# Feed-forward token blocks of 256 columns in place of 512

## The reference, cut to what matters

```python
def _moe_ref(x, w_in, w_out):
    h = x @ w_in                                # 384 -> 2048
    g = h * (1.0 / (1.0 + np.exp(-1.702 * h)))
    return (g @ w_out).astype(np.float32)       # 2048 -> 384

def _moe2_ref(x, w_in, w_out):
    h = x @ w_in
    g = h - np.tanh(h)
    return (g @ w_out).astype(np.float32)

# reference: x is the attention's output as (3072, 384)
x = _moe_ref(x=x, **moe_kwargs)
return _moe2_ref(x=x, **moe2_kwargs)
```

## Time and profile before

| | us |
|---|---|
| median of 2 runs (1152.47 to 1153.01) | 1152.74 |
| the profiled execution | 1147.88 |
| its span, first to last instruction | 1146.1 |
| TensorE busy in the span | 1061.9 (93%) |
| DVE busy | 629.0 (55%) |
| ACT busy | 335.8 (29%) |
| POOL busy | 317.5 (28%) |

### The profile page before, as it was taken

The page is one execution under the profiler, slowest core; times in us unless marked ns, Lnnn a source line. Parts: engine busy times, 40 slices in busy tenths (PEclk is TensorE's granted clock), DMA queues, the critical chain, the costliest instruction groups (busy, mean ns, idle before and its releaser), DMA issues.

```text
span 1146.1 us, 23498 instructions
## 1 busy us (share of the span) xinstructions
PE 1061.9 (93%) x8640; PEld 913.5 (80%) x8640; DVE 629.0 (55%) x1906; ACT 335.8 (29%) x646; POOL 317.5 (28%) x460
## 2 busy tenths in 40 slices
PE   4878787888788999999999999999999999999997
PEld 4877777778787888888888888888888888888886
DVE  8999999999994433333333334333333334333332
ACT  0111111111114533333333335533333333333332
POOL 6677767776774510000000005510000000000000
PEclk9888888887888999999999999999999999999999
DMA  3222322322235500000000003300000000000000
GB/s 92 77 63 73 79 67 67 79 79 58 76 92 161 167 28 1 1 1 1 1 1 1 0 0 94 99 14 1 28 1 28 1 1 28 1 28 0 27 0 27
DMA packets 50717, 46.97 MB, mean 41 GB/s; under 512 B 24400, under 2 KB 46032, under 8 KB 50640
## 3 DMA queue, kind: packets, MB, share of 16 engines
q1 hardware_dynamic: 46544, 41.13, 12.7%
q10 hardware_dynamic: 4096, 4.72, 1.3%
HBM read 36.39 MB, written 9.44 MB: 40 GB/s over the span
## 4 chain that ended last, share of the span: by engine, by line
PE 81%; DVE 11%; issue 6%; DMA 1%; ACT 0%; SPq 0%; DVEq 0%; ACTq 0%; POOL 0%; POOLq 0%
PE bank L510 34%; PE bank L522 34%; DVE scores L791 4%; PE bank L455 4%; PE bank L421 2%; DVE sf L674 2%; PE bank L466 2%; PE bank L475 1%; PE bank L485 1%; PE bank L426 1%; DVE pf L674 1%; DVE t L674 1%; DVE k L733 1%; PE bank L440 1%; DVE sf L671 1%
## 5 line engine op out<-in xcount | busy, mean ns | idle before, releaser
L510 PE MATMUL bank<-x_hi,win_hi 128*128 128x512 f32 x576 | 225.4, 391 | 2.2 <-DVE x_lo L848 2.2
L510 PE MATMUL bank<-x_hi,win_lo 128*128 128x512 f32 x576 | 225.2, 391 | 0.0
L510 PE MATMUL bank<-x_lo,win_hi 128*128 128x512 f32 x576 | 225.0, 391 | 0.0
L522 PE MATMUL bank<-g_hi,wout_hi 128*128 128x512 f32 x576 | 224.3, 389 | 0.8 <-DVE g_lo L863 0.8
L522 PE MATMUL bank<-g_lo,wout_hi 128*128 128x512 f32 x576 | 224.1, 389 | 0.0
L522 PE MATMUL bank<-g_hi,wout_lo 128*128 128x512 f32 x576 | 224.1, 389 | 0.0
L863 DVE TENSOR_TENSOR g_lo<-g,g_hi 128x512 fp32r<-128x512 f32 x192 | 133.7, 696 | 134.2 <-ACT g_hi L634 134.2
L791 DVE COPY_PREDICATED scores<-mask,bank 128x144 f32<-128x144 int32 (+2 forms) x576 | 168.1, 292 | 3.1
L634 ACT ACTIVATE g_hi<-g 128x512 fp32r<-128x512 f32 x192 | 121.5, 633 | 149.4 <-DVE g L858 74.9
L860 DVE TENSOR_TENSOR g<-bank,sg 128x512 f32<-128x512 f32 x96 | 66.3, 691 | 176.4 <-ACT sg L630 176.4
L858 DVE TENSOR_TENSOR g<-bank,sg 128x512 f32<-128x512 f32 x96 | 66.3, 691 | 175.8 <-ACT sg L628 175.8
(11 more groups left out here) (60 smaller groups left out, 1334.3 us busy)
## 6 DMA issues: line engine op xcount, KB each, us to landing
w_raw<-w_in SPq DMA_DIRECT2D x32, 192.0 KB, 2.3
w_raw<-w_out SPq DMA_DIRECT2D x32, 192.0 KB, 2.5
alpha<-a_t SPq DMA_DIRECT2D x64, 72.0 KB, 2.1
r<-q_t SPq DMA_DIRECT2D x64, 72.0 KB, 2.3
k<-k_t SPq DMA_DIRECT2D x64, 72.0 KB, 2.1
v<-v_l SPq DMA_DIRECT2D x32, 144.0 KB, 2.2
attn_out<-y ACTq DMA_DIRECT2D x64, 72.0 KB, 2.0
x_all<-attn_out SPq DMA_DIRECT2D x6, 768.0 KB, 4.5
```

The source lines that it names most:

```text
L510: last = nc.tensor.matmul(pH[f % 2][:], win(w, f, m), x[xp][:, m, :], start=(n == 0), stop=(n == len(terms) - 1))
L522: last = nc.tensor.matmul(pO[m][:], wout(w, f, m), gp[f % 2][:], start=(f == 0 and n == 0), stop=(f == NF - 1 and n == 2))
```

## The change

The token block has 256 columns instead of 512, so there are twelve blocks per layer. Every tile of the feed-forward part that holds tokens is half as wide, and the PSUM tiles use the first half of their banks. The x loads follow the new number of blocks: block 1 is loaded after weight slice 2, block 2 after slice 3 and so on, blocks 10 and 11 after slice 11. Before, block 1 was loaded after slice 3, block 2 after slice 5 and so on.

```diff
@@ -66,7 +66,7 @@
-TB = 512
+TB = 256
 NT = TOK // TB
 TILES = NT * NF
@@ -165,8 +165,8 @@
-        pH = [bank[0], bank[1]]
-        pO = [bank[2 + m] for m in range(KC)]
+        pH = [bank[n][:, 0:TB] for n in range(2)]
+        pO = [bank[2 + m][:, 0:TB] for m in range(KC)]
@@ -222,9 +222,9 @@
             if m == 1:
-                nc.vector.tensor_copy(dst, pO[m][:]).then_inc(o_copied, 1)
+                nc.vector.tensor_copy(dst, pO[m]).then_inc(o_copied, 1)
             else:
-                nc.scalar.activation(dst, pO[m][:], ACT.Copy).then_inc(o_copied, 1)
+                nc.scalar.activation(dst, pO[m], ACT.Copy).then_inc(o_copied, 1)
@@ -298,8 +298,10 @@
             for F in range(2, NF):
                 for side in range(2):
                     load_slice(side, F)
-                if F % 2 and F // 2 < NT:
-                    load_x(F // 2)
+                if F < NT:
+                    load_x(F - 1)
+                if F == NT - 1:
+                    load_x(NT - 1)
@@ -507,7 +509,7 @@
-                    last = nc.tensor.matmul(pH[f % 2][:], win(w, f, m), x[xp][:, m, :],
+                    last = nc.tensor.matmul(pH[f % 2], win(w, f, m), x[xp][:, m, :],
...
```

More of the change, by code:

```diff
@@ L521, in down @@
                     for n, (w, gp) in enumerate(terms):
-                        last = nc.tensor.matmul(pO[m][:], wout(w, f, m), gp[f % 2][:],
+                        last = nc.tensor.matmul(pO[m], wout(w, f, m), gp[f % 2][:],
                                                 start=(f == 0 and n == 0), stop=(f == NF - 1 and n == 2))
@@ L627, in _ @@
                     if layer == 0:
-                        nc.scalar.activation(SG[f % 2][:], pH[f % 2][:], ACT.Sigmoid, scale=1.702).then_inc(sg_done, 1)
+                        nc.scalar.activation(SG[f % 2][:], pH[f % 2], ACT.Sigmoid, scale=1.702).then_inc(sg_done, 1)
                     else:
-                        nc.scalar.activation(SG[f % 2][:], pH[f % 2][:], ACT.Tanh).then_inc(sg_done, 1)
+                        nc.scalar.activation(SG[f % 2][:], pH[f % 2], ACT.Tanh).then_inc(sg_done, 1)
                     act.wait_ge(g_done, N + 1)
@@ L857, in _ @@
                     if layer == 0:
-                        nc.vector.tensor_tensor(G[f % 2][:], pH[f % 2][:], SG[f % 2][:], ALU.mult).then_inc(g_done, 1)
+                        nc.vector.tensor_tensor(G[f % 2][:], pH[f % 2], SG[f % 2][:], ALU.mult).then_inc(g_done, 1)
                     else:
-                        nc.vector.tensor_tensor(G[f % 2][:], pH[f % 2][:], SG[f % 2][:], ALU.subtract).then_inc(g_done, 1)
+                        nc.vector.tensor_tensor(G[f % 2][:], pH[f % 2], SG[f % 2][:], ALU.subtract).then_inc(g_done, 1)
                     dve.wait_ge(gh_done, N + 1)
```

## The result

The changed kernel takes 1219.76 us (two runs, 1219.54 to 1219.99) against 1152.74; the ratio is 1.0581, with a 95% interval of 1.0536 to 1.0627. The forecast was 1218 in a range from 1186 to 1254. The profiled execution took 1219.99, its span is 1217.8, against 1146.1 before: 71.7 us more.

The account below looks back on a forecast made before the run. TensorE alone was taken to set the pace, with over a microsecond of side-chain slack. 46.1 + 7.8 + 7.4 + 5.6 - 1.6 = +65.3 us on 1147.9, plus 4.9 to the median, gave 1218 us, range 1186 to 1254.

Parts of the forecast that it names:

- Step 1: Feed-forward matmuls on TensorE: one fixed gap of 13.3 ns each, so 120 ns at 256 columns, +46.1 us.
- rival A: The gap between matmuls scales with the columns: 113.3 ns each, 1189 us in all; chance 0.10.
- Rival B: Not slower: the gap vanishes at short lengths, only the load's 112 ns remains, 1153 us; chance 0.08.
- Step 2: Weight loads on TensorE: each holds the array 0.112 us, just below 0.120, and costs nothing.
- Rival C: Weight load and gap add: 125 ns per matmul, 1246 us in all; chance 0.12.
- Rival D: Loads don't overlap matmuls at this length: 0.218 us each, 1876 us in all; chance 0.03.
- Step 3: ACT and DVE side chain: remainder usable 2.12 us after the last up matmul starts; fits by 0.05 us.
- two-step rule: Two steps tied by the side chain last max(36 x 0.120, 2.23 + 17 x 0.120) = max(4.32, 4.27) us.
- Steps 4 and 5: Per block: x_lo makes product 7 late, +7.8 us; DVE's copy out of output banks delays slice 0, +7.4 us.
- Step 6: Weights being split, block 0 and last block of layer 1: 2.36 us a step against 2.16, +5.6 us.
- Step 7: Start about 1.6 us earlier, about 1.0 lost to slice 3 queued behind x, shorter end: together -1.6 us.

Follow-up runs that it names:

- experiment 10: Blocks of 128 columns, 24 per layer, x loads after the weights, otherwise the changed kernel: 3310.9 us (one run).
- experiment 5: Changed kernel (256 columns) with one more DVE operation of 192 columns before each product: 1264.5 us, ratio 1.100 to the kernel before.
- experiment 6: Kernel before (512 columns) with one more DVE operation of 192 columns before each product: 1152.9 us, ratio 1.003.
- experiment 1: Changed kernel with the split of the next block's x cut in thirds, at slices 6, 7 and 8: 1211.5 us, ratio 1.052 to the kernel before.
- experiment 2: Changed kernel with a second set of output banks for odd blocks: 1213.2 us, ratio 1.054 to the kernel before.
- experiment 3: Changed kernel with x of block 1 loaded after weight slice 3, blocks 2 to 11 after all layer 1 weights: 1211.6 us, ratio 1.052.

## Why the prediction was right, and where it was not

**Step 1, the matmul.** Right in size: 120.0 ns at 256 columns, and 173.3 at 384. The fixed gap is shown at three lengths, and rival A falls by them. One leg of the argument was wrong: attention's missing gap. Rows of the timeline at three moments within the twelve records of the earlier trace rows, each beginning with the oldest matmul that still runs:

```profile
204.67 0.57 PE L455 MATMUL bank<-r,k 48*64 48x160 f32 x5
...
204.71 0.53 PE L455 MATMUL bank<-r,k 48*64 48x160 f32 x4
...
204.81 0.47 PE L455 MATMUL bank<-r,k 48*64 48x160 f32 x4
```

The starts are 0.036 and 0.100 apart in turn. The two heads lie in two halves of the rows and run side by side, and one half has a matmul every 0.136 us: 0.85 ns per column, not 0.417. The 0.0667 was an average over both halves. These rows, which are also of another type, float32, said nothing of a float32r column or its gap. So they gave no ground for 120 over 113.3 ns, and that the choice came out right is partly luck. Rival B rested on the same rows.

**Step 2, the weight load.** Right: a load holds the array for 0.112 us (experiment 10), reading it from the two load starts after a stall was sound, and its record of 0.19 is not the price. Rival C (load and gap add) is refuted by 0.120. Rival D is refuted by the interval too: load and stream in series would be 0.218. The rule that the prediction quotes beside it from the Trainium skill, "TensorE: Matmul & The Clock Gate", Part 3, doesn't hold here: loads and matmuls on the same 128 rows start 0.12 apart throughout.

**Step 3, the side chain.** Right in kind and in size. The remainder ends 2.07 after the start of the last up matmul, and where a load waits for it, it starts 0.05 to 0.06 later (experiment 5: the remainder ends at 603.81, the load starts at 603.87), which makes 2.12, the forecast. The single lengths are off by up to 0.02 and cancel. Experiment 5 shows the two-step rule, experiment 6 that it has no force at 512.

**Steps 4 and 5, slices 7 and 0.** Right in place, releaser and size, and each removed alone (experiments 1 and 2).

**Step 6, the weight loop.** Right in size for layer 2's weights (2.4 for 2.8), but it had only half of the mechanism. It let POOL's operation be longer (1.1), and the trace shows that DVE's is too: of a POOL remainder and a DVE remainder in SBUF, the one that starts second takes up to the whole overlap longer. In block 0 of the changed kernel:

```profile
378.13 0.96 DVE L850 TENSOR_TENSOR x_lo<-x_all,x_hi 128x768 fp32r<-128x768 f32 x1 [0.31 <-ACT x_hi L618]
378.59 1.37 POOL L332 TENSOR_TENSOR win_lo<-w_raw,win_hi 128x384 fp32r<-128x384 f32 x1 [1.32 <-ACT win_hi L581]
...
382.04 1.01 POOL L332 TENSOR_TENSOR wout_lo<-w_raw,wout_hi 128x384 fp32r<-128x384 f32 x1
382.14 1.20 DVE L865 TENSOR_TENSOR g_lo<-g,g_hi 128x256 fp32r<-128x256 f32 x1 [0.48 <-ACT g_hi L636]
```

POOL takes 1.37 instead of 1.00 behind x_lo, and g_lo 1.20 instead of 0.43 behind POOL. So g_lo, the end of a chain without slack, is late in the steps in which weights are split. What share of the stalls of blocks 0, 11 and 12 this is, no run separates.

**Step 7, block 0 and the start: mis-sized.** "The six more x transfers (12 of half the size) pass before they are needed" looked at who needs x, not at who stands behind it. Issued one per slice in steps half as long, they double the rate at which x competes with the weights. I had 3.8 us with the weight loop; it was 10.8, and experiment 3 takes 8.3 off the 13.8. The start came out 1.4 us late instead of 1.6 early: 2.2 because attention itself ended later in this execution, and x_lo of block 0 took 1.67 us in place of 0.96. The first is chance: over all kept profiles the last attention matmul starts between 349.5 and 355.8, in code that no edit touched. The second is POOL, which had begun a remainder first, as in step 6; experiments 2, 3 and 5, which have the same overlap, have the same 1.67:

```profile
352.78 0.99 POOL L332 TENSOR_TENSOR wout_lo<-w_raw,wout_hi 128x384 fp32r<-128x384 f32 x1
...
352.92 1.67 DVE L850 TENSOR_TENSOR x_lo<-x_all,x_hi 128x768 fp32r<-128x768 f32 x1 [0.56 <-ACT x_hi L618]
```

**The sum and the hit.** The sum was 6.4 us short in the span, and the distance of 4.9 us between the profiled execution and the median of before, which I added to it, filled most of that: after the change the two coincide. So that the forecast missed by only 1.7 us is partly luck; the terms together are good to about 6 us, of which 2.2 is the chance end of attention. The distance itself was chance too: the later runs of the kernel before have medians of 1149.7 to 1150.9, 2 to 3 us below the 1152.7 that it was taken from.

## What to carry to other kernels

Before halving a matmul, count three prices: the gap that comes with each one, the time a weight load holds the array (from two load starts after a stall, not from the record's length), and the slack of the chain of other engines, which doesn't halve, since ACT and DVE operations keep a fixed part (here 0.38 to 0.43 us each at 256 columns, 0.60 to 0.69 at 512). When the last one is gone, everything that used to be free (a copy out of a bank, a conversion in one piece, a transfer queued before another) shows as a stall; cut such work into pieces that fit the idle time left in a step, or give it another buffer. A transfer that nobody waits for still costs, if it stands ahead of one that somebody waits for.

## What the runs showed of the hardware

- The gap between matmuls at the upper clock is 13.3 ns with float32r operands (226.7, 173.3 and 120.0 ns at 512, 384 and 256 columns), 8 with half the weight columns, 12 for a pair of matmuls on half the rows each, 2.5 with bfloat16 (0.109 and 0.2156 us at 256 and 512). I had not expected the operand type to decide it.
- With 128 columns the interval is 0.112 at the upper level, set by the load, and the chip then kept the lower level to the end of the feed-forward part, while its matmul records showed it busy throughout. With 256 columns and more it kept the upper one. The feed-forward matmuls span 2950 us there, 3.4 times the 859 of 256 columns.
- Two stalls of over 2 us in block 0 (2.4 and 2.2) were each followed by some 3 us of matmuls 0.213 apart, i.e. at the lower clock level; its stalls of up to 1.2 us were not. It is no fixed rule: the stalls of 2.5 and 2.2 us of experiment 2 and of 3.3 and 3.2 us of experiment 5 were followed by the lower level, the one of 2.4 us of experiment 1 (at 361.4) was not.
- An elementwise operation of DVE with both inputs in SBUF and one of POOL don't run at the same speed side by side: the one that starts second is longer (x_lo 1.67 for 0.96, g_lo 1.20 for 0.43, POOL 1.37 for 1.00; 2.18 for 1.01 behind the x_lo of 1.76 us in block 0 of the kernel before).
